# A fused attention, cosine-gated layer and expert layer: repacked queries, keys and values, another prologue order, and changed ends

## The reference

```
h = np.maximum(xc[mask] @ w1[e], 0.0)        # 512 -> 1024
y[mask] = gate_w[mask, None] * (h @ w2[e])   # 1024 -> 512
out[do_compute] = xc + y
```

## Time and profile before

| | |
|---|---|
| time, median of 3 (lowest, highest) | 840.38 us (839.9, 841.39) |
| the profiled execution: its time, its span | 839.99 us, 838.4 us |
| PE busy | 818.1 us, 98% of the span |
| DVE, ACT, POOL busy | 508.7, 466.4, 75.7 us |
| moved by DMA | 93.87 MB, mean 112 GB/s |

### The profile page before, as it was taken

How to read it: one execution, slowest core, us unless ns; L and a number is a source line. 1 busy time by engine, 2 the same in 40 slices (tenths; PEclk the granted TensorE clock), 3 DMA queues, 4 the chain that set the end, 5 groups by cost and what they waited for, 6 DMA issues and landing times.

```text
span 838.4 us, 19569 instructions
## 1 busy us (share of the span) xinstructions
PE 818.1 (98%) x8178; PEld 727.1 (87%) x8178; DVE 508.7 (61%) x1021; ACT 466.4 (56%) x824; POOL 75.7 (9%) x96
## 2 busy tenths in 40 slices
PE   5999999999999999999999999999999999999997
PEld 4888888888888888888888898889898988999996
DVE  3588755565565556555655655564644878855663
ACT  2588765566565557555655555565545656444441
POOL 0200000010001001000100010001121332211000
PEclk9999999999999999999999999999999999999999
DMA  7761032103220421221031103202004699566300
GB/s 290 267 209 65 27 113 65 64 27 114 69 65 22 140 68 61 83 96 64 26 114 65 64 26 139 65 2 76 2 13 175 219 382 367 198 229 249 120 15 27
DMA packets 42864, 93.87 MB, mean 112 GB/s; under 512 B 9487, under 2 KB 9487, under 8 KB 42768
## 3 DMA queue, kind: packets, MB, share of 16 engines
q1 hardware_dynamic: 39280, 86.23, 28.9%
q0 software_dynamic: 3488, 6.30, 2.2%
HBM read 78.16 MB, written 17.00 MB: 113 GB/s over the span
## 4 chain that ended last, share of the span: by engine, by line
PE 90%; DMA 4%; DVE 3%; issue 1%; ACT 1%; SPq 1%; POOL 0%; POOLq 0%; DVEq 0%
PE h_ps L891 31%; PE y_ps L905 31%; PE h_ps L1051 8%; PE y_ps L1065 8%; PE s_ps L773 2%; PE s_ps L810 2%; DMA raw_a<-w 2%; PE turn L833 1%; PE turn L823 1%; PE turn L788 1%; DMA k_pre<-qk 1%; PE s_ps L845 1%; DMA lists<-pairs,place 1%; PE turn L932 0%; PE y_ps L810 0%
## 5 line engine op out<-in xcount | busy, mean ns | idle before, releaser
L891 PE MATMUL h_ps<-xT_hi,in_hi 128*128 128x384 f32 x512 | 178.4, 348 | 0.0
L891 PE MATMUL h_ps<-xT_hi,in_lo 128*128 128x384 f32 x512 | 172.4, 337 | 0.0
L891 PE MATMUL h_ps<-xT_lo,in_hi 128*128 128x384 f32 x512 | 171.7, 335 | 0.0
L905 PE MATMUL y_ps<-out_hi,g_hi 128*128 128x512 f32 x384 | 150.9, 393 | 0.9 <-DVE g_lo L1448 0.7
L905 PE MATMUL y_ps<-out_hi,g_lo 128*128 128x512 f32 x384 | 151.6, 395 | 0.0
L905 PE MATMUL y_ps<-out_lo,g_hi 128*128 128x512 f32 x384 | 151.3, 394 | 0.0
L1145 ACT ACTIVATE hs<-h_ps 128x384 f32<-128x384 f32 x128 | 62.3, 487 | 154.0 <-PE h_ps L891 153.7
L1442 DVE TENSOR_SCALAR whole<-us 128x384 f32<-128x384 f32 x128 | 46.0, 359 | 132.2 <-ACT us L1146 130.4
L1169 ACT ACTIVATE us<-us 128x384 f32<-128x384 f32 x128 | 67.3, 525 | 68.4 <-DVE us L1444 68.0
L891 PEld LDWEIGHTS h_ps<-xT_hi,in_hi 128*128 128x128 f32 x512 | 96.4, 188 | 3.2
L891 PEld LDWEIGHTS h_ps<-xT_lo,in_hi 128*128 128x128 f32 x512 | 96.5, 188 | 2.3
(11 more groups left out here) (209 smaller groups left out, 1285.4 us busy)
## 6 DMA issues: line engine op xcount, KB each, us to landing
raw_a<-w SPq DMA_DIRECT2D x32, 512.0 KB, 7.6
raw_b<-w SPq DMA_DIRECT2D x32, 512.0 KB, 7.6
k_sb<-qk SPq DMA_DIRECT2D x22, 512.0 KB, 4.5
v_sb<-v SPq DMA_DIRECT2D x22, 512.0 KB, 3.7
x_mid<-x SPq DMA_DIRECT2D x24, 256.0 KB, 4.4
out<-x SPq DMA_DIRECT2D x24, 256.0 KB, 5.0
q_sb<-qk SPq DMA_DIRECT2D x22, 256.0 KB, 3.0
in_raw<-w_in SPq DMA_DIRECT2D x4, 1024.0 KB, 6.2
```

The costliest lines, as they stand in the source:

```text
L891: last = pe.matmul(h_ps[:, f % 2, 0:BN], w[:, dc, f * P:(f + 1) * P], x[:, half, dc, :], start=(n == 0), stop=(n == 3 * DC - 1))
L905: last = pe.matmul(y_ps[:, j, :], g[:, f % RING, j * P:(j + 1) * P], w[:, f, :], start=(f == 0 and n == 0), stop=(f == FT - 1 and n == 2))
```

## The change

- **Rows of 2 KB.** Queries and keys of a tile are stored as three rows of 512 numbers per partition, values as two, and a tile needs two transfers (768 KB and 512 KB) where it needed three.
- **The prologue.** 64 small identity products at the start for 32. PE does `probs` 2 before `values` 1, and `x` 0 before `values` 2 as before; the 3 fillers stand behind `x` 1. `values` of tile 1 goes to `s_ps`, so that it waits for `s_ps` to be free and not for DVE to have taken `values` 0. DVE takes `sum` 1 before `values` 0, `sum` 2 before `values` 1, and `x` 0 before `values` 2. ACT takes the columns of `w_in` earlier, the first one ahead of `x` 0. SP issues `out_raw` only when two tiles' `values` are done.
- **Main loop.** ACT copies `us` first and signals it with a semaphore of its own (`us_done`), for which `fraction` waits. In the last step of the last block, `g_hi` and `g_lo` of the step before are made ahead of that step's copies.
- **Routing of the last block.** The 4 fillers go; half of the turning products of expert 0 stand ahead of `ranks`.
- **Experts.** The low part of the last quarter of w1 of expert 0 is made behind the first `eg_lo`. w2 of expert 1 is loaded at the start of the last block, when its buffer's attention tiles are done. Where `second_half` is skipped, PE's wait is replaced by one product of 9 columns.

```diff
-PROLOGUE_PE = [("scores", 0), ("scores", 1), ("probs", 0), ("scores", 2), ("probs", 1), ("values", 0), ("values", 1),
-               ("probs", 2), ("x", 0), ("values", 2), ("x", 1), ("x", 2)]
-PROLOGUE_ACT = [("exp", 0), ("probs", 0), ("exp", 1), ("probs", 1), ("exp", 2), ("probs", 2), ("x", 0), ("x", 1),
-                ("w_in", 0), ("x", 2), ("w_in", 1), ("w_in", 2)]
-PROLOGUE_DVE = [("scores", 0), ("scores", 1), ("sum", 0), ("scores", 2), ("values", 0), ("sum", 1), ("values", 1),
-                ("sum", 2), ("values", 2), ("x", 0), ("x", 1), ("x", 2)]
+PROLOGUE_PE = [("scores", 0), ("scores", 1), ("probs", 0), ("scores", 2), ("probs", 1), ("values", 0), ("probs", 2),
+               ("values", 1), ("x", 0), ("values", 2), ("x", 1), ("x", 2)]
+PROLOGUE_ACT = [("exp", 0), ("probs", 0), ("exp", 1), ("probs", 1), ("exp", 2), ("probs", 2), ("w_in", 0), ("x", 0), ("w_in", 1),
+                ("x", 1), ("x", 2), ("w_in", 2)]
+PROLOGUE_DVE = [("scores", 0), ("scores", 1), ("sum", 0), ("scores", 2), ("sum", 1), ("values", 0), ("sum", 2),
+                ("values", 1), ("x", 0), ("values", 2), ("x", 1), ("x", 2)]
...
-        def values_bank(B):
-            return y_ps[:, 1:3, 0:HP * HD] if is_first(B) else s_ps[:, :, 0:HP * HD]
+        def values_bank(B, j):
+            return y_ps[:, 1:3, 0:HP * HD] if is_first(B) and j != 1 else s_ps[:, :, 0:HP * HD]
...
-                sp.dma_start(to_q, qk[bass.ds(tile, 1), :, 0:HP * P].rearrange("a p n -> (a p) n")).then_inc(ld, 16)
-                sp.dma_start(to_k, qk[bass.ds(tile, 1), :, HP * P:].rearrange("a p n -> (a p) n")).then_inc(ld, 16)
+                sp.dma_start(to, qk[tile, :, :, :].rearrange("r p n -> p r n")).then_inc(ld, 16)
...
             load_in(0)
+            sp.wait_ge(v_full, 2)
             load_out(0)
...
+                    sp.wait_ge(t_full, use(B - 1, "x", BT - 1) + 1)
+                    carry(sp)
+                    load_raw2(1, 1, lambda w: w[1, :, :])
...
                     if is_first(B):
-                        wait(pe, v_free, j)
+                        wait(pe, s_free, (0, 3, 3)[j])
+                        wait(pe, v_free, (0, 0, 1)[j])
...
-            for n in range(32):
+            for n in range(64):
...
-                if (step, j) == ("values", BT - 1):
+                if (step, j) == ("x", 1):
                     keep_running(turn[:, 0, 0:P], 3)
...
-            keep_running(y_ps[:, 1, 0:P], 4)
+            pe.wait_ge(xg_ld[0], 32)
+            gathered_rows(0)
             pe.wait_ge(route_step, ROUTE * (BLOCKS - 1) + CHOSEN)
             ranks().then_inc(last_ranks_full, 1)
+            gathered_rows(1)
...
                 with pe.If(rows < P + 1):
-                    pe.wait_ge(ey_full, 2 * s + 1)
-                    pe.sem_inc(ey_full, 1)
+                    pe.matmul(y_ps[0:32, 1, 0:NL], ident[:, 0:32], ident[:, 0:NL], start=True, stop=True).then_inc(ey_full, 1)
...
-                act.activation(hs[:, f % 2, :], h_ps[:, f % 2, 0:BN], ACT.Copy)
                 act.activation(us[:, f % 2, :], h_ps[:, f % 2, 0:BN], ACT.Copy, scale=1.0 / TWO_PI,
-                               bias=0.25).then_inc(h_free, 1)
+                               bias=0.25).then_inc(us_done, 1)
+                act.activation(hs[:, f % 2, :], h_ps[:, f % 2, 0:BN], ACT.Copy).then_inc(h_free, 1)
...
-                    chain_first = f == 1 and not has_router(B)
+                    chain_first = (f == 1 and not has_router(B)) or (f == FT - 1 and is_last(B))
...
             w1_low(0, 0, 2)
-            w1_low(0, 0, 3)
...
+                    if isinstance(s, int) and s == 0 and g == 0:
+                        w1_low(0, 0, 3)
```

More of the change, by code:

```diff
@@ L283, in program @@
         h_free = sem("h_free")
+        us_done = sem("us_done")
         whole_done = sem("whole_done")
@@ L552, in run, with load_raw2 @@
                     load_list(0, list_ld[0])
+            def load_raw2(s, par, expert):
+                for n in range(4):
+                    sp.dma_start(raw2[par][:, 2 * n:2 * n + 2, :],
+                                 expert(w2)[2 * n * P:(2 * n + 2) * P, :].rearrange("(c p) d -> p c d", p=P)
+                                 ).then_inc(raw2_ld[par][n], 16)
             for B in range(BLOCKS):
@@ L577, in load_raw @@
                     sp.wait_ge(xg_ld[1], rows_landed(1))
-                for n in range(4):
-                    sp.dma_start(raw2[par][:, 2 * n:2 * n + 2, :],
-                                 expert(w2)[2 * n * P:(2 * n + 2) * P, :].rearrange("(c p) d -> p c d", p=P)
-                                 ).then_inc(raw2_ld[par][n], 16)
+                else:
+                    wait(sp, w2lo_done, 4 * (s - 1))
+                    load_raw2(s, par, expert)
             sp.wait_ge(h_full, BLOCKS * FT)
@@ L766, in attend @@
                     to = scores_banks(B, j)
-                    queries = q_pre[:, j - 1, :, :] if ahead else q_sb[:, :, :]
-                    windows = k_pre[:, j - 1, :, :, :] if ahead else k_sb[:, :, :, :]
+                    given = qk_pre[:, j - 1, :, :] if ahead else qk_sb[:, :, :]
+                    queries, windows = queries_of(given), keys_of(given)
                     for hp in range(HP):
@@ L803, in attend @@
                     carry(pe)
-                    to = values_bank(B)
-                    windows = v_pre[:, j - 1, :, :] if ahead else v_sb[:, :, :]
+                    to = values_bank(B, j)
+                    windows = values_of(v_pre[:, j - 1, :, :] if ahead else v_sb[:, :, :])
                     for hp in range(HP):
@@ L963, in _, with gathered_rows @@
             last_logits(2)
-            keep_running(y_ps[:, 1, 0:P], 4)
+            def gathered_rows(i):
+                for dc in (2 * i, 2 * i + 1):
+                    for a in range(2):
+                        c = (dc % 2) * SLOT + a * P
+                        pe.matmul(s_ps[:, i, c:c + P], xg[0][:, a, dc * P:(dc + 1) * P], ident[:, :],
+                                  start=(dc % 2 == 0 and a == 0), stop=False)
+            pe.wait_ge(xg_ld[0], 32)
+            gathered_rows(0)
             pe.wait_ge(route_step, ROUTE * (BLOCKS - 1) + CHOSEN)
             ranks().then_inc(last_ranks_full, 1)
-            pe.wait_ge(xg_ld[0], 32)
-            for dc in range(DC):
-                for a in range(2):
-                    c = (dc % 2) * SLOT + a * P
-                    pe.matmul(s_ps[:, dc // 2, c:c + P], xg[0][:, a, dc * P:(dc + 1) * P], ident[:, :],
-                              start=(dc % 2 == 0 and a == 0), stop=False)
+            gathered_rows(1)
             def last_rows(part, i, j, ends):
@@ L1191, in run @@
                         g_high(B, f - 1)
-                    elif has_router(B):
+                    elif f == 0 and has_router(B):
                         g_high(B - 1, FT - 1)
@@ L1632, with in_rows @@
     values = windows_of(v, mem_v).transpose(0, 3, 2, 5, 4, 1, 6).reshape(tiles, P, -1)
-    given = {"qk": np.concatenate([queries, keys], axis=2), "v": values, "w_in": moe_w_in, "w_out": moe_w_out,
+    def in_rows(a):
+        return a.reshape(tiles, P, -1, 512).transpose(0, 2, 1, 3)
+    given = {"qk": in_rows(np.concatenate([queries, keys], axis=2)), "v": in_rows(values), "w_in": moe_w_in, "w_out": moe_w_out,
              "w_skip": moe2_w_skip, "w_gate": moe2_w_gate, "w1": moe2_w1, "w2": moe2_w2}
```

57 lines of the change are left out of this document (28 added, 29 removed).

## The result

The changed kernel takes 835.59 us (median of 6, 834.75 to 836.32) against 840.57 for the kernel before in the same measurement: ratio 0.9945, 95% interval 0.9931 to 0.9959. It is faster, by 5.0 us where 7.6 were forecast, and the time lies 2.8 above the predicted 832.8 and 0.2 outside the range. The profiled execution took 835.24, with a span of 833.6 (before: 838.4). From the start of slot 2 on the two spans agree to the last digit: 144.63 us in both.

What follows compares the result with a forecast made beforehand. PE was taken as busy throughout the middle, so gains lay at the two ends: -4.5 - 0.2 - 0.5 - 0.3 - 2.1 = -7.6 us from 839.99 gives 832.4, stated as a median of 832.8; range 830.4 to 835.4.

Steps and rivals of the forecast that it cites:

- The sum of the prologue: Start of the kernel: first `up` reached at 25.2 instead of 29.73, -4.5 us.
- the stop of 1.38: Prologue: PE's stop in `values` 1 with nothing to wait for, 1.38 us, counted as gone within the -4.5.
- a rival at 0.24: Prologue: the 1.38 us stop stays, costing the same wherever it falls, by instruction blocks in `values` 0; 834.2; chance 0.24.
- The clock rose sooner: Prologue: PE's clock is up by about 20 us, so `up` starts at 23.3, 1.9 us sooner; 830.9; chance 0.25.
- Their chain moves with the last block, by 0.5 us, and by nothing else: Tail: expert 1's rows come only 0.5 us sooner; beyond that -0.3 is kept, with a new `xg_b` wait of about 1.2.
- Main loop: Block 0: -0.2 us from copying `us` first; last step: -0.5 from making `g_lo` ahead of the copies.
- The 0.69 of the earlier trace: Slot 0: moving the low part behind `eg_lo` frees 0.69 us at 661.44, which does not reach the end.
- Slots 0 and 1: Expert slots: stops of 0.30, 0.72 and 0.64 go, with 0.16 overlap each: -2.1 us, or -1.7 if the branch.
- Rows of 2 KB: First loads: three tiles' queries and keys might land 0.5 us sooner; 0 taken, -0.5 kept for the range.

Runs made afterwards that it cites:

- e11: As e3, but with the old prologue order on PE, ACT and DVE and the old bank for `values` 1: 836.65 us, ratio 0.996.
- e16: Changed kernel with the queries and keys of tile 0 loaded in two transfers instead of one: 835.62 us, ratio 0.995.
- e2: Changed kernel with 32 small products at the start instead of 64: 834.31 us, ratio 0.9929.
- e9: As e3, with 76 small products ahead of the prologue instead of 64: 833.92 us, ratio 0.9932.
- e10: As e9, with four filler products ahead of the turning of expert 1's rows: 833.19 us, ratio 0.992.
- e13: As e3, with 12 small products behind the last `down` and four fillers ahead of the turning of expert 1's rows: 832.49 us, ratio 0.9923.
- e17: As e8, with 15 small products replacing three prologue fillers, and four fillers ahead of the turning of expert 1's rows: 831.62 us, ratio 0.9907.
- e15: As e14, with the queries and keys of tile 0 loaded in two transfers instead of one: 833.0 us, ratio 0.9918.
- e14: As e13, without the 64 small products ahead of the prologue: 832.36 us, ratio 0.9914.
- e7: As e3, with the old wait at the skipped second half put back: 832.96 us, ratio 0.9922.
- e8: As e3, without the 64 small products ahead of the prologue: 831.45 us, ratio 0.9902.
- e18: The kernel of e8 once more, as the control of e17: 831.49 us, ratio 0.9908.
- e3: Changed kernel with the load of the first quarter of `w_in` issued only when scores 2 are done: 831.67 us, ratio 0.9903.
- e12: The kernel of e3 once more, as a control: 833.15 us, ratio 0.9919.

## Why the prediction was wrong

- **The sum of the prologue left the stop out** (the step "It comes from the stop of 1.38, the two waits for DVE, and the gap ahead of `x` 2"). This is the step that failed: it counted the stop as gone, though nothing in the new order removes it. In its place the profile has two stops, 1.42 and 2.70, 4.1 us in all. The rest of that chain was right: e11 shows the three gaps for DVE, 0.99, 1.08 and 0.97, and 3.5 us for the order. The stop has nothing to do with the order. It stands behind PE's record 703 in the kernel before and in the changed kernel alike, in `values` 1 there and in `values` 0 here, and the other one behind record 447. The Trainium skill (Runtime: NRT & Kernel Launch, Instruction fetch mechanics) has instructions fetched in blocks of 256; the trace agrees, 703 - 447 = 256. By that rule I had put the stop into `values` 0, as a rival at 0.24: it is there. The same page has the fetch hidden behind the pace at which instructions are issued. Here it is not: PE goes on 2.3 to 2.7 us after its 16 KB packet began, and 256 records of small products take 2.3 us (1.17 for 128), so a packet that comes only a little late makes PE stop. What makes one stop 0.7 and another 3.1 us long, and why the one at 447 is missing in some executions, stays open. The price was too small too, 1.4 in the rival, 4.1 in the profiled execution and 0.9 to 4.2 in the others.
- **The clock rose sooner**, the other rival, at 0.25. `x` 1 ended 3.5 us behind the forecast (23.8 for 20.3), the first `up` began 1.6 behind it (26.8 for 25.2 on the forecast's scale; 1.9 by the table): between the two, the clock gave back 1.9. The rivals were priced as alternatives, and both came true at once. The four profiles of this prologue (26.81, 23.71, 25.93, and 24.55 in e16) have their mean at 25.25, close to the forecast (24.9 in the timeline). That is luck: two errors stand against each other.
- **"Their chain moves with the last block, by 0.5 us, and by nothing else"** is the step that failed in the tail. The list was issued 17.56 us behind the last `down` for 18.00 before, and took 3.36 us for 1.9 to land; from its issue to that of the second gather there are 5.70 us for 4.19. The cause is shown: in the twenty profiles the list takes 2.7 to 3.4 us where a packet of PE's instructions comes 0.7 to 1.2 us behind its issue, and 1.8 to 1.9 where none does: in the kernel before, where the packet is moved away (e2, e9, e10, e13, e17), or where it happens to come sooner with the same program on PE (e15 against e14). That the two share the DMA engines is my reading of it. The wait for `xg_b` became 2.2 for 1.2. In five of twelve profiles the clock fell behind that wait, which cost 1.6 more; not in the one above.
- **Main loop: a term too small.** -1.33 for -0.7. Matched product by product, 0.5 had come by 42 us, in block 0, where 0.2 was forecast; another 0.5 came with the stop of the earlier trace rows, which is gone, as forecast; and 0.3 in small amounts between, for which no term stood. One wait of 0.3 for `g_lo` is left, in block 0.
- **The 0.69 of the earlier trace rows** that was to go in slot 0 went: `up_slot` begins at 655.96 without a wait for `eg_lo`. As forecast, it does not reach the end, since `xg_b` binds there.
- **Slots 0 and 1: -1.60 for -2.1.** ACT does not wait for w1 of expert 2 any more, which was right. The stops of 0.30 and 0.64 at the skipped halves were sized as wholly gone, with 0.16 of overlap each; each leaves 0.16 for the product that takes its place, and e7 puts the replaced wait at 0.22 and 0.17 where 0.46 was forecast for the first.
- **Rows of 2 KB:** I took 0 and kept a gain of 0.5 for the range. The first scores start 0.58 later (5.83 for 5.25), by the one transfer (e16), and it is covered.

The version to keep is the changed kernel with `in_raw` behind the third tile's scores and without the small products: 831.45 and 831.49 (e8, e18), 0.9902 and 0.9908 of the kernel before. e17 does not beat it, and with the small products (e3, e12: 0.9903 and 0.9919) it is not clearly slower.

## What to carry to other kernels

Where an engine runs many short instructions while the loads are at their busiest, its own program is a load too: a stop called "issue" that stands at a fixed count of the engine's instructions stays whatever the order of the work, so it belongs in the sum, and adding "free" instructions in front moves the work that it hits. When an edit changes how many instructions an engine has, look for small transfers on a chain (a list, a scatter) that its instruction packets may meet. And where a stretch ends on a chain of transfers, ask what the next one behind it is before counting a microsecond won: here `xg_b`, then `xg_a`.

## What the runs showed of the hardware that was not expected

- All stops of PE called "issue" in the first 25 us of twenty profiles stand behind record 447, 703 or 959 (products and weight loads), 0.7 to 3.1 us long, and PE goes on 2.3 to 2.7 us after a 16 KB packet of instructions began.
- With a 16 KB packet of instructions of PE beside them, 2 KB list loads landed after 2.7 to 3.4 us and not 1.9, and one issue of SP took 1.69 us for 0.47.
- Behind stops of 1.50 to 2.55 us at the higher clock level PE was at the lower one in 6 of 6 profiles, behind stops of 0.8 to 1.4 us in none of 5.
- The unchanged prologue differed by 3.1 us between two executions (first `up` at 26.81 and 23.71), the work of the main loop by 0.1.
- With one 768 KB transfer the first tile's scores began at 5.5 to 5.9, with two of 256 and 512 KB at 5.1 to 5.25.
- After an idle time of 2.1 to 2.3 us, behind the last block, PE worked at the lower clock level for about 3 us in 5 of 12 profiles, and kept the higher one in the other 7.
